# Decay masks copied out of SBUF lanes on two queues, and 14 instead of 24 empty products

## The reference, cut to what matters

```python
B, H, S, D = 2, 8, 768, 64                  # lam: one decay factor for each head
for b in range(S // 64):                    # linear attention with decay, in blocks
    intra = (qb @ kb.T) * Dmask             # Dmask[h, i, j] = lam[h] ** (i - j) for i >= j, else 0
    out_b = intra @ vb + (qb * lam ** (pos + 1)) @ kv_state
    kv_state = lam ** 64 * kv_state + (kb * lam ** (63 - pos)).T @ vb
x = out as [B, S, H * D]
u = x + real(fft(fft(x, axis=1), axis=2))   # Fourier mixing, then a 512-2048-512 MLP with layer norm
x = u + relu(norm(u) @ w_ch1) @ w_ch2
result = x + relu(norm(x) * g_ln @ w_ch1') @ w_ch2'      # a second MLP of the same shape
```

## Time and profile before

| what | value |
|---|---|
| median of 3 runs | 603.95 us (602.69 to 604.63) |
| the profiled execution's own time | 602.97 us |
| its span in the profile | 600.7 us |
| PE busy | 584.0 us, 97% |
| DVE, ACT, POOL busy | 359.4, 234.6, 157.6 us |
| DMA engines, mean busy share from 15 us to 75 us | about 0.9 and over |

### The profile page before, as it was taken

One profiled execution on the slowest core, in us unless ns is written; L12 is line 12 of the kernel. 1 busy time (PEld: TensorE's weight loads), 2 busy tenths in 40 slices (PEclk: granted clock), 3 DMA queues, 4 the chain that ended last, 5 costly groups with the idle time before them and its releaser, 6 DMA issues.

```text
span 600.7 us, 10765 instructions
## 1 busy us (share of the span) xinstructions
PE 584.0 (97%) x4063; PEld 395.6 (66%) x4063; DVE 359.4 (60%) x637; ACT 234.6 (39%) x476; POOL 157.6 (26%) x141
## 2 busy tenths in 40 slices
PE   8999998999999999999989998999999999999997
PEld 4899765776666666666656565666666666666663
DVE  2277859997776776656769677653355543422223
ACT  0232366644564233423546654334223333323231
POOL 0635883244350002004173640240000600000000
PEclk9799999999999999999999999999999999999999
DMA  7999990000032734733216562012100123000001
GB/s 223 375 348 387 388 258 15 1 19 2 1 71 55 208 106 126 166 78 106 70 36 113 141 151 71 1 36 53 36 1 1 29 60 106 36 36 2 0 1 71
DMA packets 78516, 59.87 MB, mean 100 GB/s; under 512 B 39418, under 2 KB 65666, under 8 KB 77060
## 3 DMA queue, kind: packets, MB, share of 16 engines
q1 hardware_dynamic: 76260, 54.49, 31.7%
q10 hardware_dynamic: 1728, 3.15, 1.4%
q0 software_dynamic: 480, 1.57, 1.0%
HBM read 43.73 MB, written 6.30 MB: 83 GB/s over the span
## 4 chain that ended last, share of the span: by engine, by line
PE 77%; DVE 9%; DMA 3%; ACT 3%; issue 3%; POOL 2%; SPq 1%; DVEq 0%; ACTq 0%; POOLq 0%
PE bank L620 34%; PE bank L600 30%; PE bank L452 3%; PE bank L501 3%; PE bank L417 2%; PE bank L447 2%; DMA arena<-w 2%; DVE arena L1226 1%; DVE arena L1084 1%; DMA arena<-attn 1%; PE bank L430 1%; ACT arena L858 1%; DVE arena L1085 1%; DVE arena L1092 1%; PE bank L556 1%
## 5 line engine op out<-in xcount | busy, mean ns | idle before, releaser
L620 PE MATMUL bank<-arena 128*128 128x512 f16 x1152 | 287.4, 379 | 3.9 <-DVE arena L1234 2.3
L600 PE MATMUL bank<-arena 128*128 128x256 f16 x2016 | 259.4, 273 | 3.1 <-issue 1.8
L600 PEld LDWEIGHTS bank<-arena 128*128 128x128 f16 x2016 | 196.2, 98 | 78.2 <-DVE arena L1085 2.1
L620 PEld LDWEIGHTS bank<-arena 128*128 128x128 f16 x1152 | 112.0, 98 | 91.2 <-issue 2.8
L1226 DVE SCALAR_TENSOR_TENSOR arena<-arena 128x512 f16<-128x512 f32 x96 | 72.2, 752 | 72.8 <-ACT arena L858 72.7
L858 ACT ACTIVATE arena<-arena 128x512 f16<-128x512 f32 x96 | 60.4, 629 | 101.0 <-DVE arena L1267 95.6
L1261 DVE SCALAR_TENSOR_TENSOR arena<-bank,arena 128x256 f32<-128x256 f32 x48 | 20.2, 422 | 64.6 <-PE bank L600 64.5
L1445 POOL TENSOR_TENSOR arena<-arena 128x512 f32<-128x512 f32 x12 | 18.6, 1569 | 88.3 <-DVE arena L1190 88.3
L897 ACT ACTIVATE arena<-bank 128x256 f32<-128x256 f32 x48 | 18.3, 381 | 57.3 <-PE bank L600 57.3
L1202 DVE TENSOR_TENSOR arena<-arena 128x512 f16<-128x512 f32 x42 | 33.1, 795 | 10.8 <-ACT arena L842 10.8
L1267 DVE SCALAR_TENSOR_TENSOR arena<-bank,arena 128x256 f32<-128x256 f32 x48 | 20.2, 421 | 27.8 <-PE bank L600 27.8
(11 more groups left out here) (103 smaller groups left out, 521.0 us busy)
## 6 DMA issues: line engine op xcount, KB each, us to landing
arena<-w SPq DMA_DIRECT2D x48, 256.0 KB, 4.7
arena<-w SPq DMA_DIRECT2D x24, 512.0 KB, 4.0
arena<-attn SPq DMA_DIRECT2D x10, 1024.0 KB, 8.2
x_dram<-arena ACTq DMA_DIRECT2D x12, 256.0 KB, 6.2
out<-arena SPq DMA_DIRECT2D x12, 256.0 KB, 2.1
arena<-attn SPq DMA_DIRECT2D x4, 512.0 KB, 4.2
arena<-c SPq DMA_DIRECT2D x1, 1153.5 KB, 11.4
arena<-arena SPq DMA_TRANSPOSE x35, 3.1
```

Of the source, the lines that this page charges most:

```text
L600: last = nc.tensor.matmul(bank_, wst[:, i, wx, w, kt, :], xs[s % 2][:, x, ux, :, kt, :], start=not started and k == 0, stop=k == 5, skip_g ...
L620: last = nc.tensor.matmul(ops[t][:], hT[n % 2][:, half, hx, t * P:(t + 1) * P], wdn[:, i, wx, half * DM:(half + 1) * DM], start=first and ...
```

## The change

The table of powers is built in all 128 partitions, 16 partitions (`LANES`) with the same head's values, instead of in 8. The masks are read straight out of SBUF: for each head one DMA, which takes its 128 shifted rows of 512 bytes from one partition (partition 16 h for head h). SP issues the four even heads and ACT the four odd ones, each after the wait for `pow_step`. SP issues v of block 0 before that wait. The table still goes to DRAM (for `powrow`), now behind the masks, then k of block 0, and only then SP waits for `pow_out`. The masks have a semaphore for each queue, 64 each. ACT's first instruction waits for the table and the four issues. The number of empty products between the first scores and the first `rows` is 14 instead of 24.

```diff
+LANES = P // H
-WARM_BEFORE, WARM_BETWEEN = 11, 24
+WARM_BEFORE, WARM_BETWEEN = 11, 14
+        mask_in = [sem(f"mask_in{par}") for par in range(2)]
+        def toeplitz(h):
+            v = powers[LANES * h:LANES * h + 1, 1:P + 1]
+            return bass.AP(v.tensor, v.offset, [v.ap[0], [1, P], [1, P]])
...
-            sp.dma_start(powers[0:H, P - 1:P], lam.rearrange("(h o) -> h o", o=1)).then_inc(lam_in, 16)
+            sp.dma_start(powers[:, P - 1:P], bass.AP(lam.tensor, 0, [[1, H], [0, LANES], [1, 1]])).then_inc(lam_in, 16)
...
+            sp.dma_start(flat[0][:, 3072:4096], attn_in[0, :, 3072:4096]).then_inc(v_first, 16)
             sp.wait_ge(pow_step, 9)
-            sp.dma_start(pow_dram, powers[0:H, :]).then_inc(pow_out, 16)
-            sp.dma_start(flat[0][:, 3072:4096], attn_in[0, :, 3072:4096]).then_inc(v_first, 16)
+            for pair in range(PAIRS):
+                sp.dma_start(DT[:, 0, pair, :], toeplitz(2 * pair)).then_inc(mask_in[0], 16)
+            sp.dma_start(pow_dram, powers[0:P:LANES, :]).then_inc(pow_out, 16)
+            sp.dma_start(flat[0][:, 2048:3072], attn_in[0, :, 2048:3072]).then_inc(k_first, 16)
             sp.wait_ge(pow_out, 16)
-            for par in range(2):
-                sp.dma_start(DT[:, par, :, :],
-                             bass.AP(pow_dram.tensor, 1 + par * PITCH, [[1, P], [2 * PITCH, PAIRS], [1, P]])
-                             ).then_inc(mask_in, 16)
-            sp.dma_start(flat[0][:, 2048:3072], attn_in[0, :, 2048:3072]).then_inc(k_first, 16)
...
-            act.wait_ge(lam_in, 16)
+            act.wait_ge(pow_step, 9)
+            for pair in range(PAIRS):
+                act.dma_start(DT[:, 1, pair, :], toeplitz(2 * pair + 1)).then_inc(mask_in[1], 16)
...
-            nc.vector.memset(powers[0:H, P:P + 1], 1.0).then_inc(pow_step, 1)
+            nc.vector.memset(powers[:, P:P + 1], 1.0).then_inc(pow_step, 1)
...
-                nc.vector.tensor_scalar(powers[0:H, P - 2 * n:P - n], powers[0:H, P - n:P],
+                nc.vector.tensor_scalar(powers[:, P - 2 * n:P - n], powers[:, P - n:P],
...
-            dve.wait_ge(mask_in, 32)
             for par in range(2):
+                dve.wait_ge(mask_in[par], 16 * PAIRS)
                 last = nc.vector.tensor_copy(kcol.rearrange("p (a r) -> p a r", r=2)[:, :, par], DT[:, par, :, 0])
```

More of the change, by code:

```diff
@@ L196, in build @@
         x_dram = nc.dram_tensor("x_dram", [B * S, DM], F32).ap()
-        lam_in, pow_step, pow_out, mask_in = sem("lam_in"), sem("pow_step"), sem("pow_out"), sem("mask_in")
+        lam_in, pow_step, pow_out = sem("lam_in"), sem("pow_step"), sem("pow_out")
+        mask_in = [sem(f"mask_in{par}") for par in range(2)]
         powrow_in = sem("powrow_in")
@@ L946, in _ @@
         def _(dve):
-            nc.vector.memset(powers[0:H, P:P + 1], 1.0).then_inc(pow_step, 1)
-            nc.vector.memset(powers[0:H, P + 1:PITCH], 0.0).then_inc(pow_step, 1)
+            nc.vector.memset(powers[:, P:P + 1], 1.0).then_inc(pow_step, 1)
+            nc.vector.memset(powers[:, P + 1:PITCH], 0.0).then_inc(pow_step, 1)
             dve.wait_ge(lam_in, 16)
@@ L953, in _ @@
                 dve.wait_ge(pow_step, steps)
-                nc.vector.tensor_scalar(powers[0:H, P - 2 * n:P - n], powers[0:H, P - n:P],
-                                        powers[0:H, P - n:P - n + 1], None, ALU.mult).then_inc(pow_step, 1)
+                nc.vector.tensor_scalar(powers[:, P - 2 * n:P - n], powers[:, P - n:P],
+                                        powers[:, P - n:P - n + 1], None, ALU.mult).then_inc(pow_step, 1)
                 n, steps = 2 * n, steps + 1
-            dve.wait_ge(mask_in, 32)
             for par in range(2):
+                dve.wait_ge(mask_in[par], 16 * PAIRS)
                 last = nc.vector.tensor_copy(kcol.rearrange("p (a r) -> p a r", r=2)[:, :, par], DT[:, par, :, 0])
```

## The result

The changed kernel is slower: median 612.22 us (610.57 to 614.01, 4 runs) against 603.73 (602.69 to 604.63, 4 runs), ratio 1.0142, 95% interval 1.0108 to 1.0175. The forecast was 601.9, faster. The profiled execution took 612.53 us, span 610.2, so it is 9.4 us longer in span than the one before.

A forecast was written before the change was run, and what follows sets the result against it. PE and the DMA stream run side by side and meet in block 4. The stream's 1.0 us from earlier masks and 1.03 from the refill, 2.1 won in all, turn the median 603.95 into 601.9 us; range 600.0 to 607.5.

The forecast's parts named there:

- signs of being wrong: Masks landing after 12.8, SP's `powrow` issue after 13, half clock starting after 19 us, or block 4 early without earlier mixing.
- The table and lam: Start of kernel: loading lam to 128 partitions instead of 8 costs 0.1 us; table ready at about 3.95.
- The masks: Mask DMAs at the start: last issue at 5.27 plus 5.4 us as before, landing at 10.7, 1.6 us earlier.
- The upper bound: Mask reads: each partition gives one DMA engine's rate, 27.1 GB/s; four per queue take 9.7 us, landing at 17.2.
- rival 1: Mask reads queue at their one source partition; decides from a landing at 12.8 on, slower; chance 0.20.
- The empty products: PE before the first rows: ten fewer, 2.23 us, end at 10.8, still covered by the wait for masks.
- The rival's 608.3: Total on the median if masks land at the upper bound, 17.2: +4.4 us; chance of rival 1 0.20.
- The DMA stream: SP's loads behind the masks: waiting for `pow_out` delays `powrow` and block 1; of 1.6 us won, 1.0 is kept.
- the 6.6 of the sum: Block 1's queries land 6.6 us after the masks, at 17.3 where before it was 18.3.
- the refill that was forecast: DMA queue low at 34 to 37 us (245 GB/s against 373); PE ahead by 1 us or more recovers 1.03 us.
- Two streams that meet in block 4: Attention, block 4: PE's stream and the DMA stream meet with 0.13 us slack; the later decides, 2.1 us won.
- All of it reaches the end: After block 4: all 2.1 us won reach the kernel's end, since PE and DMA stream go on with that shift.

The follow-up runs named there:

- e2: Changed kernel with lam loaded to 8 partitions only (0, 16, ..., 112) instead of 128; 609.27 us, ratio 1.0082 to the kernel before.
- e5: Changed kernel with the table in partitions 0 to 7 alone and the same eight mask reads from there; ratio 1.0229 to the kernel before.
- e6: Changed kernel with each mask read from its head's 16 partitions instead of one (mask content not right); one run, 607.53 us.
- e9: Changed kernel with the eight masks read from single partitions that lie on eight different ports; one run, 608.73 us.
- e3: Changed kernel with 44 empty products instead of 14, keeping PE busy until the masks come; ratio 1.0121 to the kernel before.
- e12: Kernel before with its masks still read from DRAM, but as eight DMAs on two queues, and 22 empty products instead of 24; ratio 1.0038 to the kernel before.
- e1: Kernel before with lam loaded and the table built in all 128 partitions, masks still by way of DRAM; ratio 1.0029 to the kernel before.
- e10: Kernel before with 14 empty products instead of 24; ratio 0.9995 to the kernel before.
- e8: Changed kernel with all rows of a mask read from one aligned 512 bytes, without the shift (masks not right); one run, 611.40 us.
- e7: Changed kernel with the eight mask DMAs reading from DRAM after the table's write, instead of from SBUF; ratio 1.0082 to the kernel before.
- e11: Kernel before with table write and masks on ACT's queue, v and k of block 0 ahead on SP's, 18 empty products; ratio 1.0091 to the kernel before.

## Why the prediction was wrong

Two of the prediction's own signs of being wrong came: the masks landed after 12.8 (17.0), and `powrow` was issued after 13 (17.17).

- **The table and lam.** I took 0.1 us, bound at 0.4, for 128 small writes instead of 8. It was 2.3: 3.62 us for lam instead of 1.35, and 2.35 at the table. The first 1 MB behind it was 1.4 us late as well (by its landing, 7.7 instead of 6.3), and PE waited 1.04 for its queries. e2 gave 2.25 us of mixing back by undoing it, 1.3 of them at the masks. What of the load costs (the 4-byte writes, or the source that is read 16 times) was not separated.
- **The masks.** This step failed most. "I take its 5.4 us": a row with the same packets from another kind of source does not price this read. It was 10.8 us from table to masks. The upper bound, one DMA engine's rate for each queue, gave a landing at 17.2; it was 17.0. That is rival 1, with the mechanism that the experiments show (e5, e6, e9), and I gave it 0.20. What I held against it was misread: the 369 GB/s from 11 to 12 us are for the most part not the mask DMA's, since k's DMA had been going since 7.43; by the packets of the trace about 260 of them are k's rows of 4 KB. That the bound's 17.2 came so near is partly luck: v was through at about 9 instead of 7.5, the table was ready at 6.23 instead of 3.95, and the two queues together moved 69 GB/s instead of 54. I also took 0.44 us for an issue; with the DMA engines held up, the last one on ACT took 2.84.
- **The empty products.** "Still covered" was right for 10.7, not for 17.0: PE stood still for 6.45 us, and the clock fell before it started again. The rival's 608.3 had no term for that. By e3 it was worth 1.2 to 1.7 us before the mixing.
- **The DMA stream.** `powrow` was issued at 17.17, right behind the masks, as the step said; POOL began on block 1's queries 7.3 us after the masks (24.31 less 17.00), near the 6.6 of the sum. The 350 GB/s from 34 to 37 us look like the refill that was forecast and are not: PE was behind, SP asked for the next keys at 39.88 instead of 33.32, and the gap had moved to 41 to 43 us, at 259 GB/s. In e12, where PE was ahead, no microsecond from 24 to 47 us was under 340 GB/s.
- **Two streams that meet in block 4.** Half right. In the changed kernel POOL ended block 4's keys at 57.03 + 1.91 = 58.94 and PE began at 59.07, the same 0.13 us. But that is no fixed wall: from block 1 to block 4 every kernel took 27.2 to 28.3 us, and 27.2 is PE's own pace there, six units of 4.53. SP issues each load when PE has ended a block, so a late PE makes late loads. e12 was ahead by 2.9 and 2.1, where the forecast said 3.1 and 2.1, but that agrees by luck: its masks came 0.6 us earlier and not 1.6, and the clock that stayed up gave the rest. That part of PE's lead is lost to the wait for keys, as the forecast had it, is borne out by e12's waits for POOL.
- **All of it reaches the end.** Wrong even where the attention was faster. e12 won 2.1 us by 64.8 and lost them, and more, by 111. In the changed kernel 0.76 us were added between mixing and MLP (PE's wait for DVE was 2.81 instead of 2.06) and 2.07 after, of which half of a dip of 3.4 us would explain 1.7, and a later wait for DVE (2.91 instead of 2.32) 0.6.

The sum with measured terms: 2.35 (lam) + 2.30 (reads) + 2.18 (half clock, and keys that come later) - 0.22 = 6.6 before the mixing, 0.76 + 2.07 behind it.

Open: what sets off the late dips of the clock. One stands near 100 us in e1, e6 and e12 only (mixing starts at 66.71, 67.94 and 64.80; before at 66.92 and e10 at 67.59 have none), and one at 373 to 387 in every profiled kernel but before and e10. Each begins where PE goes on after a pause for DVE, from 0.4 us before to 1.1 us after, at the same two places of the program. In the changed kernel this is the pause in front of the dip at 379.9:

```profile
379.74 1.33 PE L626 MATMUL bank<-arena 128*128 128x512 f16 x3 [2.91 <-DVE arena L1242]
```

Near 100 us the pauses in front of dips are 2.06 (e1, e6) and 2.82 us (e12), later 2.60 to 3.24. The pause alone does not do it: 2.06 near 100 us had no dip in before and e10, nor 2.81 in the changed kernel, nor the late pauses of before (2.32) and e10 (2.91). No run took such a dip away with all else equal. The mean clock of single executions says how much half clock there was in all, not where. It differs among executions of one kernel: beside e1 the kernel before had 1.000 in one (600.34 us), so not even the 6.8 us of its profile, 0.997 in others (604.06, 603.64) and 0.991 in one (604.41). Beside e10, its executions with 0.996 or 0.997 took 602.5 to 604.0 us and those with 0.988 took 607.1 to 609.5. Beside e12, 10 of its 17 had 0.997, about half of the half clock of the profiled one (0.994), so the 2.1 us by which e12 leads in the two profiles may be more than its usual lead.

What makes the clock fall at the start is open too: before it fell after PE had stood still for 0.92 and 0.97 us, in e1 it stayed at 1.00 after 1.54 and 0.55.

## What to carry to other kernels

A DMA that fans one SBUF partition out to all partitions goes at the rate of one port, here about 25 GB/s, whether one queue reads there (the changed kernel) or two (e5), and wherever its rows begin (e8): put the sources on different ports, or go by way of DRAM, which was faster here by 3.6 us although it adds a write and a wait. Price a new kind of access by its bounds, and let a bound that has a mechanism weigh as much as the nearest row. Before you count on an early gain, look for what it meets later; here 2.1 us won by 65 us were gone at 111. And read several executions before you price a change in one stage by two profiles.

## What the runs showed of the hardware that was not expected

- The issuing queue is held when the DMA engines are held up at the source: four issues on SP's queue took 5.8 to 6.5 us in the changed kernel, e2 and e3, 10.9 in e5, 2.9 in e6, and 1.8 with DRAM as the source (e7). All that stands behind them on that queue is late by that.
- DMA share does not tell such a stall from work: 0.71 busy at 50 GB/s (the changed kernel), 0.65 at 25 (e5), 0.80 at 181 (e6).
- One load of eight values spread to 128 partitions: 3.62 us instead of 1.35.
- An 8 KB write, first on its own queue, took 6.3 us behind loads issued earlier on the other queue (e11), against 2.5 before.
- A clock at half for 17 us cost 1.2 to 1.7 us at the end of the stage (e3), since data was late as well; a dip of 3.4 us in the dense part is estimated at 1.7, half of its length.
- The late dips begin where PE goes on after a pause of 2.06 to 3.24 us for DVE, and behind pauses as long there is none in other profiles (before, the changed kernel near 100 us, e10).
